# Sparse attention and two expert layers on one core: joint transposes of two heads' last keys, a hand-given order of the first tile, and split scores in the second tile

## What is computed

```python
# 4 batches, 8 heads, 576 queries and keys, head width 64; all float32
scores = q @ k.T / 8
thresh = max(scores, axis=-1) - tau                 # tau = 0.02
scores = where(scores >= thresh, scores, -1e9)
attn   = exp(scores - max(scores))
attn   = attn / (sum(attn) + 1e-9)
x = attn @ v                                        # heads side by side: 2304 tokens x 512
h = x @ moe_w_in                                    # 512 -> 2048
x = (h * tanh(softplus(h))) @ moe_w_out             # 2048 -> 512
g = x @ moe2_w_gate                                 # 512 -> 1536
out = (g * sigmoid(g) * (x @ moe2_w_val)) @ moe2_w_out
```

## Time and profile before

| | |
|---|---|
| median of 3 runs | 1135.1 us (1134.78 to 1136.54) |
| the profiled execution | 1134.82 us |
| its span, first to last instruction | 1133.0 us |
| PE busy | 1110.8 us (98%) |
| DVE, ACT, POOL busy | 469.7, 461.6, 501.2 us |
| transposes (L721), by the page | 688 + 32 |
| granted clock | 1.00 |
| first unit matmul, the end of the first tile's attention | 58.1 us |
| stages of the MoE begin at | 58.1, 235.6, 459.2, 705.3, 944.6 us |

### The profile page before, as it was taken

One profiled execution on the slowest core, in us unless ns is written; L12 is line 12 of the kernel. 1 busy time (PEld: TensorE's weight loads), 2 busy tenths in 40 slices (PEclk: granted clock), 3 DMA queues, 4 the chain that ended last, 5 costly groups with the idle time before them and its releaser, 6 DMA issues.

```text
span 1133.0 us, 17108 instructions
## 1 busy us (share of the span) xinstructions
PE 1110.8 (98%) x6080; PEld 916.2 (81%) x6080; DVE 469.7 (41%) x941; ACT 461.6 (41%) x818; POOL 501.2 (44%) x688
## 2 busy tenths in 40 slices
PE   5899999999999999999999999999999999999998
PEld 3598788899888898888787778887787878888887
DVE  5636675621765662007554550037455520001210
ACT  6766555445544552344333440454243312401210
POOL 5677565745654663345344570454244322400220
PEclk9999999999999999999999999999999999999999
DMA  7377677888666788655455487554443456555552
GB/s 240 131 244 264 215 247 241 278 288 280 209 212 212 238 277 278 208 196 167 134 185 158 157 271 233 197 194 141 156 163 126 161 165 214 195 190 199 187 198 100
DMA packets 94626, 230.76 MB, mean 204 GB/s; under 512 B 16208, under 2 KB 31568, under 8 KB 94544
## 3 DMA queue, kind: packets, MB, share of 16 engines
q1 hardware_dynamic: 94400, 229.68, 61.2%
q10 hardware_dynamic: 144, 0.00, 0.0%
HBM read 189.27 MB, written 40.37 MB: 203 GB/s over the span
## 4 chain that ended last, share of the span: by engine, by line
PE 92%; POOL 2%; DMA 2%; SPq 1%; ACT 1%; DVE 1%; issue 1%; ACTq 0%; DVEq 0%
PE ps_m L655 25%; PE ps_m L657 24%; PE ps_m L656 24%; PE ps_x L721 6%; PE ps_x L744 6%; PE ps_s L697 2%; PE ps_s L698 2%; PE ps_s L683 2%; DMA w_raw<-weights 1%; PE ps_m L744 1%; POOL p_t L1050 1%; POOL w_sp L1061 0%; POOL k_lo L1034 0%; DMA k_raw<-kt 0%; SPq L610 0%
## 5 line engine op out<-in xcount | busy, mean ns | idle before, releaser
L655 PE MATMUL ps_m<-x_hi,w_sp 128*128 128x512 f32 (+2 forms) x800 | 301.1, 376 | 2.4 <-ACT g_raw L867 1.3
L657 PE MATMUL ps_m<-x_hi,w_sp 128*128 128x512 f32 (+2 forms) x800 | 295.4, 369 | 0.0
L656 PE MATMUL ps_m<-x_lo,w_sp 128*128 128x512 f32 (+2 forms) x800 | 295.2, 369 | 0.0
L655 PE MATMUL ps_m<-g_hi,w_sp 128*128 128x512 f32 (+2 forms) x560 | 212.1, 379 | 0.1
L657 PE MATMUL ps_m<-g_hi,w_sp 128*128 128x512 f32 (+2 forms) x560 | 206.9, 369 | 0.0
L656 PE MATMUL ps_m<-g_lo,w_sp 128*128 128x512 f32 (+2 forms) x560 | 206.8, 369 | 0.0
L944 DVE SCALAR_TENSOR_TENSOR p_t<-ps_s,thr,p_t 128x576 f32<-128x576 f32 x144 | 116.5, 816 | 145.1 <-ACT p_t L842 130.4
L655 PEld LDWEIGHTS ps_m<-x_hi,w_sp 128*128 128x128 f32 x800 | 150.2, 188 | 31.5 <-issue 11.7
L657 PEld LDWEIGHTS ps_m<-x_hi,w_sp 128*128 128x128 f32 x800 | 150.2, 188 | 22.3
L656 PEld LDWEIGHTS ps_m<-x_lo,w_sp 128*128 128x128 f32 x800 | 150.4, 188 | 19.5
L937 DVE TENSOR_REDUCE nmax<-ps_s 128x1 f32<-128x576 f32 x144 | 107.2, 752 | 86.1 <-PE ps_s L698 73.5
(11 more groups left out here) (58 smaller groups left out, 1190.7 us busy)
## 6 DMA issues: line engine op xcount, KB each, us to landing
w_sp<-scratch SPq DMA_DIRECT2D x238, 512.0 KB, 3.3
scratch<-w_sp SPq DMA_DIRECT2D x68, 512.0 KB, 3.8
w_raw<-weights SPq DMA_DIRECT2D x102, 256.0 KB, 4.1
k_raw<-kt SPq DMA_DIRECT2D x56, 288.0 KB, 3.6
v_f<-v SPq DMA_DIRECT2D x64, 128.0 KB, 2.3
out_t<-o_sb SPq DMA_DIRECT2D x12, 256.0 KB, 3.6
k_f<-kt SPq DMA_DIRECT2D x8, 288.0 KB, 4.0
q_raw<-qt SPq DMA_DIRECT2D x8, 256.0 KB, 4.2
```

Source lines behind the costliest of these rows:

```text
L655: nc.tensor.matmul(ps, w_h, x_h, start=first, stop=False)
L656: nc.tensor.matmul(ps, w_h, x_l, start=False, stop=False)
L657: return nc.tensor.matmul(ps, w_l, x_h, start=False, stop=last)
```

## The change

It has three parts.

*Joint transposes.* In pairs whose n is a multiple of 128 from the second tile on (`joined`: n = 256, 384, 128, 512), the last 64 keys of both heads are turned together. For the odd head k is loaded with its last 64 keys first (`keys_of`; the host lays kt out with 512 keys repeated behind the 576), and the slots of `p_t` are dealt so that a block of the even head and the same block of the odd head are neighbours (`slots`, 12 slots). The last 64 columns of one and the first 64 of the next then form one 128 x 128 block. The last turn of such a pair covers all its blocks: n columns in place of 2n. In `values`, one product with `v_rest` (128 keys x 128 columns, two 64 x 64 blocks of v on the diagonal, zeros elsewhere) takes the place of the last key chunk's two; it comes first. A slot of a joined pair comes free with that last turn.

*The first tile's order.* `FIRST_TILE` gives, for each engine, the kinds of the steps of the first tile's attention in order, one letter each; the planner must follow it. The v loads come behind the q and k loads in the planner's order of steps.

*Split scores in the second tile.* `WHOLE_TILES` is 1.

```diff
-P_SLOTS = 10
+P_SLOTS = 12
...
+ALL_PAIRS = PAIRS * len(PIECES)
+ALONE_PAIRS = PAIRS * (LAST_OF[0] + 1)
+
+
+def joined(J):
+
+
+    return J >= ALONE_PAIRS and queries(2 * J) % P == 0
...
+    if joined(J):
+        turns = [turn for turn in turns if turn[1] != (KC - 1,)] + [(range(blocks_of(J)), (KC - 1,))]
     return turns
 
 
-ALL_PAIRS = PAIRS * len(PIECES)
-ALONE_PAIRS = PAIRS * (LAST_OF[0] + 1)
+def rest(J, i):
+
+    return joined(J) and i == len(turns_of(J)) - 1
+
+
+def columns(J, i):
+
+    group, keys = turns_of(J)[i]
+    return queries(2 * J) if rest(J, i) else P * len(group) * len(keys)
...
+def slots():
+
+
+    place, before, holds, pair = [], [], {}, 0
+    for J in range(ALL_PAIRS):
+        n = blocks_of(J)
+        for b in range(n):
+            slot = 2 * (pair + b % (n // 2)) + b // (n // 2) if joined(J) else 2 * pair + b
+            slot %= P_SLOTS
+            before.append(holds.get(slot, -1))
+            holds[slot] = len(place)
+            place.append(slot)
+        pair += (n + 1) // 2
+    return place, before
+
+
+SLOT, HELD = slots()
+
+
+def keys_of(H):
+
+    return slice(SEQ - DH, 2 * SEQ - DH) if joined(H // 2) and H % 2 else slice(0, SEQ)
...
-WHOLE_TILES = 2
+WHOLE_TILES = 1
...
+FIRST_TILE = {
+    "PE": ({"s": "scores", "t": "tpose", "v": "values"},
+           "sssssstttsstttsstvtvtstsvvtvststtttsvsvvtttstsvttvtstsvvvtvtttvttttvvvvv"),
+    "ACT": ({"q": "q_scaled", "e": "exp", "c": "p_copy", "h": "x_high", "w": "w_high"},
+           "qqeewwqeewqweeqccceeccqceeccqceechccececcqceecccceechcceeccccchcccwwcwh"),
+    "DVE": ({"r": "rowmax", "m": "mask", "i": "recip", "l": "x_low"},
+           "rrmmirirmmirirmmririmmirirmmrirmimirlrmimriirmmirirmmilrirmmiill"),
+    "POOL": ({"t": "thresh", "e": "eps", "n": "norm", "w": "w_low"},
+           "tteettnenenttweentntenentntwewtetnewntetnenetntneenttneentnteennwww"),
+    "SP": ({"q": "load_qk", "v": "load_v", "w": "load"},
+           "qqqqwwwvvvwqqqvwvqwvwvv"),
+}
...
-            add("SP", 0.8, 2, ("load_v", H), (("values", before // 2, parts(before // 2) - 1) if before >= 0 else None, 0.1))
+            v_used = ("values", before // 2, parts(before // 2) - 1) if before >= 0 else None
...
+                add("SP", 0.8, 2, ("load_v", H), (v_used, 0.1))
...
+            add("SP", 0.8, 2, ("load_v", H), (v_used, 0.1))
...
-                kept = ("tpose",) + last_turn(C - P_SLOTS) if C >= P_SLOTS else None
+                kept = ("tpose",) + last_turn(HELD[C]) if HELD[C] >= 0 else None
...
-                    if names[k[0]][turn[k[0]]] != k:
+                    if names[k[0]][turn[k[0]]] != k or fixed[e][0:1] not in ([], [k[0]]):
...
+            del fixed[e][0:1]
...
+        v_rest, _ = sb("v_rest", [P, SLOTS // 2, P])
...
+            return x_bank(USE0[J] + i)[:, 0:columns(J, i)].rearrange("p (c q) -> p c q", c=len(turns_of(J)[i][1]))
+
+        def p_place(J, i):
+
             group, keys = turns_of(J)[i]
-            return x_bank(USE0[J] + i)[:, 0:len(keys) * len(group) * P].rearrange("p (c q) -> p c q", c=len(keys))
+            first = 0 if rest(J, i) else P * group[0]
+            return p_of(J)[:, keys[0]:keys[-1] + 1, first:first + columns(J, i) // len(keys)]
...
-                    sp.dma_start(k_f[:, slot, :], kt[head]).then_inc(k_f_loaded[slot], 16)
+                    sp.dma_start(k_f[:, slot, :], kt[head, :, keys_of(H)]).then_inc(k_f_loaded[slot], 16)
...
-                sp.dma_start(v_f[DH:P, slot, KC - 1, :], v[head, DH:P, KC - 1]).then_inc(v_f_loaded[slot], 16)
+                to = v_f[DH:P, slot, KC - 1, :]
+                rows = slice(DH, P)
+                if joined(H // 2):
+                    rows = slice(H % 2 * DH, (H % 2 + 1) * DH)
+                    to = v_rest[rows, slot // 2, rows]
+                sp.dma_start(to, v[head, rows, KC - 1]).then_inc(v_f_loaded[slot], 16)
...
+                blocks = range(blocks_of(J) // 2) if rest(J, i) else group
                 for c, key in enumerate(keys):
-                    for at, b in enumerate(group):
-                        p = p_t[:, (FIRST[J] + b) % P_SLOTS, KEY0[key]:KEY0[key] + P]
-                        last = nc.tensor.transpose(to[:, c, at * P:(at + 1) * P], p, ident)
+                    for at, b in enumerate(blocks):
+                        first = SEQ * SLOT[FIRST[J] + b]
+                        if rest(J, i):
+                            first += SEQ - DH
+                        elif joined(J):
+                            first += P * key + (DH if b >= blocks_of(J) // 2 else 0)
+                        else:
+                            first += KEY0[key]
+                        last = nc.tensor.transpose(to[:, c, at * P:(at + 1) * P], p_row[:, first:first + P], ident)
...
+                if joined(J):
+                    nc.tensor.matmul(to[:, 0:n], v_rest[:, J % 2, :], p[:, KC - 1, 0:n], start=True, stop=False)
+                    keys = range(KC - 1)
                 for key in keys:
                     for e in range(2):
                         last = nc.tensor.matmul(to[e * DH:(e + 1) * DH, 0:n], v_f[:, (2 * J + e) % SLOTS, key, :],
-                                                p[:, key, e * n:(e + 1) * n], start=key == 0, stop=key == KC - 1)
+                                                p[:, key, e * n:(e + 1) * n], start=key == 0 and not joined(J), stop=key == keys[-1] and part == parts(J) - 1)
...
-                slot = C % P_SLOTS
+                slot = SLOT[C]
                 act.wait_ge(max_ready, C + 1)
-                if C >= P_SLOTS:
-                    J, i = last_turn(C - P_SLOTS)
+                if HELD[C] >= 0:
+                    J, i = last_turn(HELD[C])
                     act.wait_ge(t_filled, TURN0[J] + i + 1)
                 act.activation(halves(p_t[:, slot, :]), s_banks(C), ACT.Exp, bias=nmax[:, slot:slot + 1]).then_inc(e_ready, 1)
 
...
+            dve.memset(v_rest[0:DH, :, DH:P], 0.0)
+            dve.memset(v_rest[DH:P, :, 0:DH], 0.0)
...
-        "kt": twice(inputs["k"].transpose(0, 1, 3, 2).reshape(heads, DH, SEQ)),
+        "kt": twice(np.concatenate([kt, kt[:, :, :SEQ - DH]], axis=2)),
```

More of the change, by code:

```diff
@@ L288, in attention @@
             for i, (group, keys) in enumerate(turns):
-                cols = P * len(group) * len(keys)
-                add("PE", 0.1075 * len(group) * len(keys), 1 if alone else 0, ("tpose", J, i),
+                cols = columns(J, i)
+                add("PE", 0.1075 * cols / P, 1 if alone else 0, ("tpose", J, i),
                     (("norm", FIRST[J] + group[-1]), near), (self.x_free(USE0[J] + i), near))
@@ L416, in order @@
         out, last_pe = [], None
+        fixed = {e: [kinds[letter] for letter in letters] for e, (kinds, letters) in FIRST_TILE.items()}
         while len(out) < len(self.step):
@@ L483, in build @@
         p_t, _ = sb("p_t", [P, P_SLOTS, SEQ])
+        p_row = p_t.rearrange("p s k -> p (s k)")
         p_f, _ = sb("p_f", [P, KC, 2 * BANK])
@@ L599, in load_qk @@
                     sp.wait_ge(s_filled, last_chunk(H - 2) + 1)
-                sp.dma_start(k_raw[:, slot, :], kt[head]).then_inc(k_loaded[slot], 16)
+                sp.dma_start(k_raw[:, slot, :], kt[head, :, keys_of(H)]).then_inc(k_loaded[slot], 16)
                 if split(H) >= 2:
@@ L844, in p_copy @@
             def p_copy(J, i):
-                group, keys = turns_of(J)[i]
                 before = J - (2 if J < ALONE_PAIRS else 1)
@@ L849, in p_copy @@
                 act.wait_ge(t_filled, TURN0[J] + i + 1)
-                to = p_of(J)[:, keys[0]:keys[-1] + 1, P * group[0]:P * (group[-1] + 1)]
-                act.activation(to, turned(J, i), ACT.Copy).then_inc(p_copied_scalar, 1)
+                act.activation(p_place(J, i), turned(J, i), ACT.Copy).then_inc(p_copied_scalar, 1)
             def x_high(t, j):
@@ L956, in p_copy @@
                 dve.wait_ge(t_filled, TURN0[J] + i + 1)
-                to = p_of(J)[:, keys[0]:keys[-1] + 1, P * group[0]:P * (group[-1] + 1)]
-                dve.tensor_copy(to, turned(J, i)).then_inc(p_copied_vector, 1)
+                dve.tensor_copy(p_place(J, i), turned(J, i)).then_inc(p_copied_vector, 1)
             def x_high(t, j):
@@ L1037, in thresh @@
             def thresh(C):
-                slot = slice(C % P_SLOTS, C % P_SLOTS + 1)
+                slot = slice(SLOT[C], SLOT[C] + 1)
                 pool.wait_ge(max_ready, C + 1)
@@ L1118 @@
     heads = BATCH * HEADS
+    kt = inputs["k"].transpose(0, 1, 3, 2).reshape(heads, DH, SEQ)
     v = inputs["v"].reshape(heads, SEQ, DH)
```

## The result

The changed kernel takes 1129.1 us (median of 4 runs, 1127.3 to 1133.0) where the kernel before, timed beside it, takes 1135.8: ratio 0.9941, 95% interval 0.9921 to 0.9961. It is 6.7 us faster; 11.7 were forecast, and 1129.1 lies 0.6 us outside the range.

What follows compares the result with a forecast made beforehand. PE work after the MoE part's first matmul at 58.1 us, and when that part starts, were taken to bound it. From 1134.8, 4.4 + 5.9 + 2.1 - 0.8 = 11.6 gave 1123.2, stated as 1123.4; range 1118.5 to 1128.5.

Steps and rivals of the forecast that it cites:

- Joint transposes, 4.4 us: MoE stages of tiles 0, 1 and 3: 40 transposes fewer at 0.109 us each take 4.4 us off PE.
- the zero that was chosen between -4.6 and +9: Values of joined pairs: the 128-wide product costs what two 64-wide ones do; ends 4.6 us gained, 9 us lost.
- I price it at nothing: Joined pairs free slots only at the joint turn; units between were to cover this, so no cost.
- The first tile, 2.1 us: First tile's new order: fifth chunk 0.6 us earlier, plus half of 3.2 us of short waits; ends 0 and 3.8.
- Split scores, 5.9 us off PE: Scores of tile 1, 28 chunks in tile 0's MoE stage: 5.9 us less PE work; ends 3.0 and 7.5.
- After: 24 x 0.53 + 4 x 1.06 = 17.0: Tile 1's split scores: 24 one-head chunks at 0.53 us and 4 two-head chunks at 1.06 take PE 17.0 us.
- the 0.2 that I added to the balance: Split scores: the stage's busy-time balance gave 5.7 us; 5.9 was taken since lone chunks prevail.
- New waits, 0.8 us: Tile 0's MoE stage: norms queue behind k_low on POOL, costing PE 0.8 us; ends -1.5 and +5.
- a ring of seven slots as cover: SP's loads wait along behind those of later heads; seven slots, some 12 us, were to cover this.
- The first, POOL and DVE in each other's way mildly: Tile 0's MoE stage: POOL and DVE slow each other, price 3 to 5 us, time 1127; chance 0.15.
- The second, POOL as the bound: POOL bounds 66:218, 161 us of work for PE's 146; 15 us of waits, time 1137.5; chance 0.04.
- rival 4: All goes well: scores give 7.5, first tile 3.8, the stage's idle 1.5 goes; time 1117.9, chance 0.06.

Runs made afterwards that it cites:

- the lists alone: The kernel before with only the first tile's step order fixed and the v loads behind the q and k loads; 1131.4 us.
- the change with longer loads: The changed kernel with the planner's load times raised: w_high 6.0 instead of 3.0, k_high 5.0 instead of 2.4, q_high 5.2 instead of 2.6; 1119.4 us.
- the split alone: The kernel before with only split scores in the second tile added; 1139.2 us, ratio 1.0036.
- that of the v loads: The kernel before with the v loads behind the q and k loads, without the first tile's fixed step order; 1134.8 us.
- joint alone: The kernel before with only joint transposes (12 slots) added; 1131.4 us, ratio 0.9967.
- before, longer loads: The kernel before with the planner's load times raised to w_high 6.0, k_high 5.0, q_high 5.2, and nothing of the change; 1137.5 us.
- the change, still longer loads: The changed kernel with the planner's load times raised further: w_high 9.0, k_high 7.5, q_high 7.7; 1135.5 us.

## Why the prediction was right or wrong

**What bounds the kernel**: right. PE work removed behind the first tile and the start of the MoE part are what counted, and every difference is one of PE's work, waits or clock.

**Joint transposes, 4.4 us**: right within the noise. 4.2 alone (2.4 to 5.1 by the interval), 4.8 in the three stages of its profile less 0.8. There are 680 transposes, as said. The joint product costs the zero that was chosen between -4.6 and +9. "I price it at nothing" for the later release of slots was up to 0.8 us too low: the norm at 671 us.

**The first tile, 2.1 us**: the size right, by luck, and by another path than the sum had it. The traces with these lists have the first unit matmul between 54.7 and 56.1 us, 2.0 to 3.4 earlier (55.3 in the changed kernel, 56.0 with the lists alone). PE did not start 1 us earlier: the first keys landed at the same time,

```profile
5.56 2.29 PE L757 MATMUL ps_s<-k_f,q_f 64*128 64x288 f32 x8 [5.56 <-DMA k_f<-kt]
...
10.81 1.32 ACT L974 ACTIVATE w_sp<-w_raw 128x512 fp32r<-128x512 f32 x2 [1.39 <-DMA w_raw<-weights]
...
14.12 2.29 PE L757 MATMUL ps_s<-k_f,q_f 64*128 64x288 f32 x8 [2.19 <-DVE p_t L1026]
```

but the first weights ended ACT's wait at 10.8 instead of 13.8, and the fifth chunk started at 14.1 (forecast 15.4, before 16.0): 1.9 us gained there, where the sum had 0.6. Behind it only 0.9 us was gained, where the sum had half of 3.2: PE's idle time fell by 2.1 (37.8 busy of 42.1 before, 38.9 of 41.2 now), but its busy time rose by 1.2, for which no row shows a cause. The two errors nearly cancel.

**Split scores, 5.9 us off PE**: too high; 4.2. The terms that were off are "After: 24 x 0.53 + 4 x 1.06 = 17.0", too low, and the 0.2 that I added to the balance. The whole chunks cost what the balance said: 174.5 busy less 119.7, 14.4 (132 transposes) and 18.0 leaves 22.4. With the split the same subtraction leaves 18.1 of the 170.2: 1.1 us more than the 17.0. The price of a split chunk between units was right (ten such chunks of one head in the change with longer loads cost 0.53 to 0.57 each, read as in the earlier trace rows), so the 1.1 us is elsewhere, and where stays open; that it is waits too short to show is my reading.

**New waits, 0.8 us**: this is the step on which the forecast fell. They came to 6.1 us in the profiled execution (5.1 instead of 1.8, 3.1 instead of 1.3, 1.3 instead of 0.4), 5.3 of the 5.7 us by which the median missed; the split's 1.7 adds to that, the first tile takes 0.7 off, and the 0.6 left over is inside the noise, the more so as the waits are read from one execution. The 3.1 us of the clock come on top in the profiled execution alone. The prediction looked for the waits on POOL, by its share of busy time, and took ACT for covered at 57% because it was not full. It had said of SP that loads "wait along", with a ring of seven slots as cover; it never asked what is queued on ACT behind a k_high or a w_high whose load is late. At 63 us that was a mish behind a k_high, a new step; at 242 a mish behind a w_high that stood there before and whose load came 1.9 us later. Moving these steps by their planned load times took 9.7 us off. The added steps were priced by their length, when the price was their place.

**The rivals.** The first, POOL and DVE in each other's way mildly (1127), came nearest. It has a small part in the cause: the wait at 212 us, with the 0.5 us by which it grew, and the first tile of the split alone are of its kind. The larger waits, for a mish, are not. The second, POOL as the bound, is refuted: in the change with longer loads POOL is busy 139.2 of 171.2 us, about as full as in the changed kernel, and PE idles 1.0. The rule of the Trainium skill beside it (SBUF — State Buffer, "two separate sides") is that VectorE instructions with two SBUF inputs and GpSimd's that read SBUF take the port pair in turn. DVE's w_low, a two-input instruction, in the stage of tile 0's MoE, before and in the changed kernel:

```profile
L973 DVE TENSOR_TENSOR w_sp<-w_raw,w_sp 128x512 fp32r<-128x512 f32 x32 | 28.0, 875 | 29.7 <-ACT w_sp L892 29.4
...
L1053 DVE TENSOR_TENSOR w_sp<-w_raw,w_sp 128x512 fp32r<-128x512 f32 x32 | 34.4, 1076 | 17.7 <-ACT w_sp L974 17.6
```

Its mean rises from 0.88 to 1.08 us, its median from 0.72 to 1.13, with POOL busy for 140.2 of 177.9 us instead of 113.2 of 177.5. The trace agrees that DVE's instructions get longer beside a busy POOL; the rival's price, which reckons each as a stop of POOL for its whole length, would have made 1137.5. A slower version did exist, the split alone with 1139.2, in the main by a late load and by ACT's order, and for about 1.5 us by q_low and k_low in the first tile.

**The range** reached 1128.5, with new waits of up to 5 us among its ends. Waits of 6.1 together with a split that gave 4.2 lie just outside it. Its other end, 1118.5, was said to be halfway to rival 4; that rival stands at 1117.9, so it is nearly all the way.

## What to carry to other kernels

When a change adds steps that need a load to an engine with a fixed order, list what is queued behind each of them on that engine, and ask how late the load may be; an engine that is half idle can still hold up the one that is full. A planner's guess for a load's time is a tuning parameter with two sides: too short puts waits ahead of urgent steps (here 9.7 us), too long starves the consumers (16 us). Try a part that removes work from the bound engine again after the waits are mended: the split scores cost 3.6 us in the kernel before, were worth nothing beside the lists and the joint pairs, and gained 3.0 us once the waits were gone.

## What the runs showed that was not expected

The granted clock fell to half for some 3.4 us at a time around single waits of PE, inside a kernel that is 98% busy. All such stretches in the traces, that of the v loads and the last two microseconds of each kernel left out:

| kernel | stretch, us | PE's wait ahead of it | ends at |
|---|---|---|---|
| the change | 212.4 to 215.9 | 2.0 us | 212.3 |
| the change | 243.1 to 246.6 | 3.1 us | 242.4 |
| joint alone | 34.3 to 37.8 | 2.9 us | 33.5 |
| split alone | 67.3 to 74.1 | 3.7 us | 68.6 |
| split alone | 251.6 to 255.0 | 3.2 us | 250.4 |
| before, longer loads | 58.3 to 61.7 | 2.2 us | 56.6 |
| the change, still longer loads | 95.8 to 99.3 | 2.3 us | 95.2 |

Each stands at a wait of 2.0 us or more, one already begins inside it, and one is twice as long as the others. But not every such wait has one: those of 3.6 us at 16.0 (the kernel before), 3.5 at 15.4 (joint alone), 4.1 at 16.5 (split alone), 2.2 at 14.1 (the change) and 2.4 at 83.3 (still longer loads) have none. So the length of a wait does not tell by itself, and a wait of 3 us behind the first tile can cost some 1.5 us more than itself.

A load of 256 KB took 8.2 us from issue to landing at the start of tile 1's MoE, where the DMA view of 225 to 240 us shows q1's packets taking 94.6% of the 16 engines' time; the median of such loads is 4.5 us. That share does not explain it: with the lists alone it is 98.4% in the same window, and the load ahead of the mish was used 6.4 us after its issue.

What stays open: why that load is 1.9 us later in the changed kernel, how the 3.9 us of k_high and q_high divide, and whether another value of the planner's times does better than 1119.4.
